# Output products of the first expert in 512-token tiles from batch 1 on, with the last 64 tokens of each batch gathered in DRAM

## What is computed

```
p_packed = sm_attn(p, k, v)                # 32 packed queries per head
out      = sm_attn(q, p_packed, p_packed)  # 576 tokens per batch
x        = out as (4608, 512)
# first expert
xn  = x / sqrt(mean(x*x) + 1e-6) * rms_g
x   = (silu(xn @ w_gate) * (xn @ w_val)) @ w_out       # d_ff 1536
# second expert
h   = x @ w_in
out = (max(h, 0) + alpha * min(h, 0)) @ w_out2         # d_ff 2048
```

## Time and profile before

| | |
|---|---|
| time, median of 3 runs | 1554.76 us (1554.55 to 1554.98) |
| the profiled execution | 1554.32 us |
| its span in the trace | 1552.5 us |
| TensorE busy (matmul) | 1539.6 us, 99% of the span |
| TensorE clock | 0.998 of full |
| VectorE / ScalarE / GpSimd busy | 728.0 / 446.4 / 196.0 us |
| first stage | to 764.8 us; one batch takes 92.3 us |
| second stage | 764.8 to 1552.5 us |

### The profile page before, as it was taken

One profiled execution on the slowest core, in us unless ns is written; L12 is line 12 of the kernel. 1 busy time (PEld: TensorE's weight loads), 2 busy tenths in 40 slices (PEclk: granted clock), 3 DMA queues, 4 the chain that ended last, 5 costly groups with the idle time before them and its releaser, 6 DMA issues.

```text
span 1552.5 us, 25676 instructions
## 1 busy us (share of the span) xinstructions
PE 1539.6 (99%) x10324; PEld 1318.5 (85%) x10324; DVE 728.0 (47%) x1281; ACT 446.4 (29%) x847; POOL 196.0 (13%) x186
## 2 busy tenths in 40 slices
PE   8999999999999999999999999999999999999999
PEld 3889889898988989889988888888888888888887
DVE  5765554645555564655443333333343333333333
ACT  4445344444534444342211111111111111111111
POOL 2700000000000000008551002020201002020000
PEclk9999999999999999999999999999999999999999
DMA  9302111021210302003400001010100000010000
GB/s 354 108 19 79 47 52 61 14 80 46 79 47 13 98 17 77 16 32 136 152 1 28 27 10 44 0 54 0 53 1 27 27 18 36 0 54 0 27 0 27
DMA packets 42738, 76.16 MB, mean 49 GB/s; under 512 B 2208, under 2 KB 19616, under 8 KB 42656
## 3 DMA queue, kind: packets, MB, share of 16 engines
q1 hardware_dynamic: 37760, 66.08, 12.6%
q10 hardware_dynamic: 4896, 8.92, 1.5%
HBM read 56.11 MB, written 18.87 MB: 48 GB/s over the span
## 4 chain that ended last, share of the span: by engine, by line
PE 96%; DVE 3%; ACT 1%; issue 1%; POOL 0%; DVEq 0%; POOLq 0%; ACTq 0%
PE psum L597 30%; PE psum L598 29%; PE psum L599 29%; PE psum L733 3%; PE psum L695 1%; PE psum L635 1%; PE psum L650 1%; PE psum L833 1%; PE psum L683 0%; PE psum L620 0%; PE psum L702 0%; DVE act_sb L1244 0%; DVE h_lo L1247 0%; DVE e L1117 0%; DVE e L1102 0%
## 5 line engine op out<-in xcount | busy, mean ns | idle before, releaser
L1280 DVE TENSOR_TENSOR h_lo<-g,h_hi 128x512 fp32r<-128x512 f32 x144 | 107.4, 746 | 470.3 <-ACT h_hi L1028 470.3
L1028 ACT CAST h_hi<-g 128x512 fp32r<-128x512 f32 x144 | 89.4, 621 | 633.3 <-PE psum L599 598.9
L597 PE MATMUL psum<-an_hi,m_hi 128*128 128x288 f32 x768 | 237.0, 309 | 2.9 <-DVE act_sb L1244 1.4
L597 PE MATMUL psum<-h_hi,ow_hi 128*128 128x288 f32 x768 | 231.6, 302 | 0.6 <-DVE h_lo L1247 0.6
L598 PE MATMUL psum<-an_hi,m_lo 128*128 128x288 f32 x768 | 225.9, 294 | 0.0
L599 PE MATMUL psum<-an_lo,m_hi 128*128 128x288 f32 x768 | 225.8, 294 | 0.0
L598 PE MATMUL psum<-h_hi,ow_lo 128*128 128x288 f32 x768 | 225.8, 294 | 0.0
L599 PE MATMUL psum<-h_lo,ow_hi 128*128 128x288 f32 x768 | 225.8, 294 | 0.0
L597 PEld LDWEIGHTS psum<-h_hi,ow_hi 128*128 128x128 f32 x768 | 144.0, 188 | 26.4 <-issue 25.4
L597 PEld LDWEIGHTS psum<-an_hi,m_hi 128*128 128x128 f32 x768 | 144.1, 188 | 25.3 <-issue 17.0
L1244 DVE TENSOR_TENSOR act_sb<-act_sb,psum 128x288 f32<-128x288 f32 x192 | 85.9, 447 | 168.7 <-PE psum L599 157.2
(11 more groups left out here) (141 smaller groups left out, 2388.7 us busy)
## 6 DMA issues: line engine op xcount, KB each, us to landing
k_sb<-k_t SPq DMA_DIRECT2D x16, 576.0 KB, 5.1
q_sb<-q_t SPq DMA_DIRECT2D x8, 1152.0 KB, 8.7
y_mid<-y_sb SPq DMA_DIRECT2D x16, 576.0 KB, 3.5
xs_raw<-y_mid SPq DMA_DIRECT2D x9, 1024.0 KB, 5.1
out_t<-o_sb ACTq DMA_DIRECT2D x34, 256.0 KB, 2.0
v_sb<-v_s SPq DMA_DIRECT2D x8, 1024.0 KB, 6.6
gv_sb<-w_gv SPq DMA_DIRECT2D x4, 1536.0 KB, 18.8
w_raw_front<-w SPq DMA_DIRECT2D x2, 2560.0 KB, 12.6
```

The costliest lines, as they stand in the source:

```text
L597: nc.tensor.matmul(dst, w_hi, hi, start=start, stop=False)
L1028: nc.scalar.copy(h2_hi[:, f % 2, :], g32[:, f % 2, :]).then_inc(g_hi_done, 1)
L1280: nc.vector.tensor_tensor(h2_lo[:, s, :], g32[:, s, :], h2_hi[:, s, :].bitcast(F32), ALU.subtract).then_inc(g_lo_done, 1)
```

## The change

From batch 1 on a batch is one tile. The up blocks stay 288 wide, but alternate between the halves: block i (0 to 23) is chunk i // 2, half i % 2. The down products of a chunk cover its first 512 tokens at once and are made in two parts of 6 matmuls (output blocks 0, 1, then 2, 3), part by part behind the up blocks, three blocks later (`WIDE_LAG = 3`). High cast and low subtraction are done once a chunk, behind the odd block, 512 wide, in two slots. The 64 tokens that are left of each chunk (of the product in `act_sb`) go by a DMA of their own to the DRAM tensor `rest_mid`, 12 a batch, and the silu of a later odd block waits for that DMA before it writes the slot again. After batch 7 they are loaded again as a ninth tile of 512 tokens (`rest`), split and multiplied (`rest_tile`).

Batch 0 keeps its two halves; the down products of the second are 224 wide (288 less 64). The next batch's `split0` and `split1` move to the end of the tile. Outputs are copied 512 wide to `y_low` and `y_high`, which lie on attention buffers, and stored in two DMAs. SyncE's loop over the batches is unrolled, with the loads of k and v in the middle of a batch. The weight loads of the mid and back part of the second expert wait until the ninth tile is stored. The host reorders the tokens of the result.

```diff
-SLOTS = 3
-LAG = 2
+SLOTS, WIDE_SLOTS = 3, 2
+LAG, WIDE_LAG = 2, 3
...
@@ TensorE
+                for i in range(BLOCKS_OF + WIDE_LAG):
+                    if i < BLOCKS_OF:
+                        up_block(b, i, i // 2, i % 2, at)
+                    if i >= WIDE_LAG:
+                        d, part = (i - WIDE_LAG) // 2, (i - WIDE_LAG) % 2
...
+                        if part == 0:
+                            pe.wait_ge(h_lo_done, h_count(b, d, 0))
+                        down((2 * part, 2 * part + 1), ow_hi[:, d, :], ow_lo[:, d, :], h_hi[:, d % WIDE_SLOTS, :],
+                             h_lo[:, d % WIDE_SLOTS, :], y_ps, d == 0, d == NF1 - 1, out_mm, down_mm,
+                             lambda: at("ready_down", i))
...
@@ ScalarE
+                    for i in range(BLOCKS_OF):
+                        f, half = i // 2, i % 2
...
+                        act.wait_ge(gate_mm, n)
...
+                        elif half == 1 and (b > 1 or f >= WIDE_SLOTS):
...
+                            freed = (b, f - WIDE_SLOTS) if f >= WIDE_SLOTS else (b - 1, NF1 + f - WIDE_SLOTS)
+                            act.wait_ge(rest_out[s], rest_count(*freed))
+                        nc.scalar.activation(act_sb[:, s, half * HALF:(half + 1) * HALF], gate_ps,
+                                             ACT.Silu).then_inc(silu_done, 1)
+                        at("after", i)
+                        if half == 1:
+                            act.wait_ge(h32_done, n)
...
+                            nc.scalar.copy(h_hi[:, s, :], act_sb[:, s, 0:TILE]).then_inc(h_hi_done, 1)
+                        at("between", i)
...
@@ SyncE
+            def store_rest(b, f):
+                i = NF1 + f if b == 0 else 2 * f + 1
+                sp.wait_ge(h32_done, BLOCKS_OF * b + i + 1)
+                src = act_0[:, f % SLOTS, TILE - HALF:HALF] if b == 0 else act_sb[:, f % WIDE_SLOTS, TILE:SEQ]
+                sp.dma_start(rest_mid[:, f, REST * b:REST * (b + 1)], src).then_inc(rest_out[rest_slot(b, f)], 16)
...
+                else:
+                    sp.wait_ge(m_mm, NF1 // 2 * BATCH)
+                    sp.wait_ge(an_lo_done, 2 * BATCH)
+                    load_w2(0, w2_raw_front[:, 0:W2_FRONT // 2, :], 0, W2_FRONT // 2)
+                    sp.wait_ge(y_stored, 32 * (BATCH - 1))
+                    load_w2(1, w2_raw_front[:, W2_FRONT // 2:W2_FRONT, :], W2_FRONT // 2, W2_FRONT)
...
+                for f in range(NF1):
+                    store_rest(b, f)
...
+                if b < BATCH - 1:
+                    store_y(b)
```

More of the change, by code:

```diff
@@ L31 @@
 NT = TOKENS // TILE
+REST = SEQ - TILE
+BLOCKS_OF = 2 * NF1
+assert REST * BATCH == TILE and NT == BATCH + 1
 BANK = 512
@@ L61 @@
     (1, "within", 6): ["means"], (1, "between", 6): ["fold2"], (1, "between", 7): ["newton"],
-    (1, "between", 8): ["fold3"], (1, "within", 10): ["split0"], (1, "between", 10): ["fold4"],
+    (1, "between", 8): ["fold3"], (1, "between", 10): ["fold4"], (1, "after", 11): ["split0"],
+    (1, "between", 11): ["split1"],
 }
@@ L68 @@
     (1, "between", 1): ["fold0"], (1, "between", 3): ["fold1"], (1, "after", 6): ["rsqrt"], (1, "between", 6): ["fold2"],
-    (1, "between", 8): ["fold3"], (1, "between", 9): ["split0"], (1, "between", 10): ["fold4"],
+    (1, "between", 8): ["fold3"], (1, "between", 10): ["fold4"], (1, "after", 11): ["split0"],
+    (1, "between", 11): ["split1"],
 }
@@ L797, in tile @@
[L797 to L812, removed]
@@ L823, in tile @@
[L823 to L828, removed]
+                            pe.wait_ge(y_act, 2)
+                            pe.wait_ge(y_dve, 2)
+                        pe.wait_ge(ow_ready, d + 1)
@@ new lines, in first_tile @@
+                        pe.wait_ge(h_lo_done, h_count(0, d, half))
+                        width = cols.stop - cols.start
+                        down(range(KC), ow_hi[:, d, :], ow_lo[:, d, :], h_hi_0[:, d % SLOTS, 0:width],
+                             h_lo_0[:, d % SLOTS, 0:width], lambda m: y_ps(m)[:, cols], d == 0, d == NF1 - 1,
+                             out_mm if half == 1 else None, down_mm, lambda: at("ready_down", i))
+                    if f < NF1:
+                        at("between", i)
@@ L844, in _ @@
             tiles_of_a(pe, tile, beside)
+            rest_tile()
             lag = 3
@@ L1014, in _, with rest_hi, rest_tile @@
+            def rest_hi(f):
+                if f % 4 == 0:
+                    act.wait_ge(rest_in[f // 4], 16)
+                act.wait_ge(down_mm, h_count(BATCH, f, 0) - 2)
+                nc.scalar.copy(h_hi[:, f % WIDE_SLOTS, :], rest[:, f, :]).then_inc(h_hi_done, 1)
+            def rest_tile():
+                for f in range(1, NF1):
+                    rest_hi(f)
+                out_of_tile(BATCH)
             nc.scalar.preload_act_table_set("natural_log_exp_and_others")
@@ L1235, in beside, with first_tile @@
                     folded(c, int(name[4]), (0, 1) if len(name) == 5 else (int(name[-1]),))
-            def tile(b, half, at):
-                n = 2 * b + half
+            def first_tile(half, at):
                 for f in range(NF1):
-                    s = f % SLOTS
-                    at("within", f)
-                    dve.wait_ge(silu_done, NF1 * n + f + 1)
-                    dve.wait_ge(hidden_mm, NF1 * n + f + 1)
-                    nc.vector.tensor_tensor(act_sb[:, s, :], act_sb[:, s, :], val_ps, ALU.mult).then_inc(h32_done, 1)
-                    at("after", f)
-                    dve.wait_ge(h_hi_done, NF1 * n + f + 1)
-                    nc.vector.tensor_tensor(h_lo[:, s, :], act_sb[:, s, :], h_hi[:, s, :].bitcast(F32),
-                                            ALU.subtract).then_inc(h_lo_done, 1)
-                    at("between", f)
-                    if half == 0 and f == 2 and b > 0:
-                        split(b, 1)
-                dve.wait_ge(y_stored, 16 * n + 16)
-                for m in range(2):
-                    dve.wait_ge(out_mm, (KC - 1) * n + m + 1)
-                    nc.vector.tensor_copy(y_sb[:, m, :], y_ps(m)).then_inc(y_dve, 1)
-                at("end", 0)
@@ new lines, in tile @@
+            def tile(b, at):
+                if b == 0:
+                    for half in range(2):
+                        first_tile(half, at)
+                else:
+                    for i in range(BLOCKS_OF):
+                        f, half = i // 2, i % 2
+                        s, n = f % WIDE_SLOTS, BLOCKS_OF * b + i + 1
+                        dst = act_sb[:, s, half * HALF:(half + 1) * HALF]
+                        at("within", i)
+                        dve.wait_ge(silu_done, n)
+                        dve.wait_ge(hidden_mm, n)
+                        nc.vector.tensor_tensor(dst, dst, val_ps, ALU.mult).then_inc(h32_done, 1)
+                        at("after", i)
+                        if half == 1:
+                            dve.wait_ge(h_hi_done, h_count(b, f, 0))
+                            nc.vector.tensor_tensor(h_lo[:, s, :], act_sb[:, s, 0:TILE], h_hi[:, s, :].bitcast(F32),
+                                                    ALU.subtract).then_inc(h_lo_done, 1)
+                        at("between", i)
+                if b == BATCH - 1:
+                    rest_lo(0)
+                out_of_tile(b)
@@ L1258, in _, with rest_lo, rest_tile @@
+            def rest_lo(f):
+                dve.wait_ge(h_hi_done, h_count(BATCH, f, 0))
+                nc.vector.tensor_tensor(h_lo[:, f % WIDE_SLOTS, :], rest[:, f, :], h_hi[:, f % WIDE_SLOTS, :].bitcast(F32),
+                                        ALU.subtract).then_inc(h_lo_done, 1)
+            def rest_tile():
+                for f in range(1, NF1):
+                    rest_lo(f)
+                out_of_tile(BATCH)
             dve.wait_ge(consts_set, 4)
```

321 lines of the change are left out of this document (221 added, 100 removed).

## The result

| | before | changed |
|---|---|---|
| time, median (lowest to highest of 3 runs) | 1554.76 us (1554.55 to 1554.98) | 1569.16 us (1567.49 to 1570.20) |
| ratio of the runs, 95% interval | | 1.0091 [1.0068, 1.0114] |
| profiled execution / its span | 1554.32 / 1552.5 us | 1567.49 / 1565.7 us |
| one batch, batches 1 to 6 | 92.32 us | 89.37 us |
| batch 7 to the start of stage two | 78.89 us | 112.05 us (with the ninth tile) |

What follows compares the result with a forecast made beforehand. TensorE, busy 99% of the span, was taken to bound the kernel. Terms -8.3 + 10.5 + 1.8 + 1.5 + 5.0 - 1.4 = +9.1 on 1554.3 gave 1563.4, forecast as 1564 us, range 1552 to 1572.

Steps and rivals of the forecast that it cites:

- The price of the columns: Down products of all batches and the ninth tile: fewer, wider matmuls change the time by -8.3 us in sum.
- The rival that priced 512 at 0.234: Down products: 512 wide costs its columns at the 288 price, the 8.3 us gain disappears, 1572 us; chance 0.02.
- The beginning of a batch: Up blocks 2 and 3, batches 1 to 7: new waits for silu and multiply, 1.5 us each, +10.5 us.
- The exponentials ... are covered by this very wait: Beginning of a batch: the wait at up block 3 hides the exponentials of the next block but one, no added cost.
- The middle of a batch: Block 13's gate part waits for the silu of block 12, 0.3 us in batches 1 to 6, +1.8 us.
- Other tight places: Shorter down steps make just-in-time waits late: 0.2 us a batch and 0.3 for batch 0, +1.5 us.
- The stores: 64-token pieces: free in batches 0 to 6; in batch 7 queued behind weight loads, delaying block 5's silu, +5.0 us.
- the rival in which all batches queue: Stores of pieces land 2 us late in each of batches 1 to 6, 12 us more, 1570 to 1576 us; chance 0.13.
- The stall that goes: Last half of batch 7: TensorE's wait for a low subtraction beside GpSimd's weight split disappears, -1.4 us.
- only the columns count: Whole kernel: short waits don't appear and stores land early, 1545 us; with partial waits up to 1551, chance 0.12.

Runs made afterwards that it cites:

- all three edits: Changed kernel with fold5 early, exponentials one block later, and batch 7's weight loads behind pieces 1 and 5: 1550.57 us, ratio 0.9968 to the kernel before.
- the exponentials alone: Changed kernel with the next batch's two exponentials one block later, fold5 left in place: 1565.85 us, ratio 1.0066 to the kernel before.

## Why the prediction was right, and where it was off

The direction and the range held, and the waits that the sum counted are in the trace where it put them. One sentence failed, about the exponentials, and one cost was never thought of, the clock behind the long wait; together they cost 4.4 us, and terms that were counted too high made up a part of it. By the forecast's own steps, against the profiled execution (1554.3 to 1567.5, +13.2 us where +9.1 were summed):

- **The price of the columns** held where rows gave it. In the ninth tile, down blocks start 2.72 us apart, 0.2267 us a matmul. The one width without a row was off: 224 wide, twelve take 1.34 us (127.11 to 128.45), 0.1117 each, where the line gave 0.1045. Batch 0 became 3.2 us shorter and not 3.6. The rival that priced 512 at 0.234 is refuted there. Inside a batch it is half right: a down part that stands alone between two up blocks takes 1.38 us, 0.230 a matmul, where two in a row take 2.72. The Trainium skill (TensorE: Matmul & The Clock Gate, Back-to-back issue gap) gives 2.5 ns over the width at 2.4 GHz for an isolated gap, and 131 ns at 512 for a sustained stream. Neither is what this trace shows, 226.7 ns at 512.
- **The beginning of a batch**: 1.5 us were summed for up blocks 2 and 3. Measured: 2.72 - 1.68 and 1.90 - 1.58, 1.4 in all. Moving `fold5` took this wait away, so its cause is shown; the edit moved ScalarE's and VectorE's part together, so the split between the two is read from the rows.
- **"The exponentials ... are covered by this very wait"** is the sentence that failed. The silu of block 4 still came late: the down part before block 5 took 1.87 us instead of 1.38, 0.5 a batch, and moving the exponentials gave 0.6. That is more than the 0.37 by which each batch was longer than forecast (89.37 against 89.0); other terms came out smaller. The slip was to let the wait at block 3 delay TensorE and not ScalarE's own chain: the silu of block 3 waits for block 3's gate part (1.15 us idle, 228.34), so table load, exponentials, wide cast and table load all start later as well.
- **The middle of a batch**: 0.3 were summed. The down part ahead of block 13 took 1.63 or 1.64 us instead of 1.38, 0.25. The silu of block 12 starts 4.71 us after that of block 11 (257.27), where 4.72 were forecast, and block 13 starts when it has ended (262.44). No experiment moves the probabilities' exponential, so this cause is read from the rows and not tested.
- **Other tight places**, 0.2 a batch: down parts take 1.38 us and not 1.36 where they stand alone, about 20 times a batch. That makes 0.4. A batch is 2.3 us longer than its columns would make it (89.37 against 92.3 - 5.3), and 2.1 are named above, so some 0.2 are left for these: something else became shorter by about as much, and it was not looked for.
- **The stores**: the place in the queue, the moment (a piece issued at S + 5.1, landed at about S + 19.8 where 20.5 to 21 were forecast) and the wait on TensorE were right; 3.9 us idle instead of 5.0. What was missing is its consequence: the block behind the wait ran at half clock, 3.01 us instead of 1.58. Together 5.5 us, and 5.6 came back when the loads were moved. Elsewhere the pieces cost nothing even when stored twice, so the rival in which all batches queue is refuted.
- **The stall that goes** went: in the changed kernel no long subtraction (the longest is 2.38 us) stopped TensorE in batch 7. That a lag of three is what protects it is shown by the lag of two, where three of them did.
- The execution profiled also reached its first up block 0.9 us later than that of before (34.49 against 33.55). In the seven experiments it is between 33.94 and 34.62, always later than in the one trace of before, and I don't know why.

So the four parts that differ from the forecast are 2.1 us in batches 1 to 6, 0.8 in batch 7, 0.4 in batch 0 and 0.9 at the start, 4.2 where 4.1 were to be found. The first two are in the main the exponentials (3.0 in six batches) and the half clock (1.4), less what the beginning of a batch, its middle and the wait for the store fell short of their terms. The last two stay open: traces with the same code there differ by 0.9 us in batch 0 (95.3 and 96.2) and by 0.7 in the start. The medians are 1.2 us further apart than the profiled executions; no trace shows where.

The rival "only the columns count" was refuted as a forecast, but it is nearly where the kernel goes once the order of work is made again: with all three edits it stands at 1550.6 us, 4.5 us under the kernel before, where that rival had 1545. In the trace batch 0 is 3.2 us shorter and six batches 4.7 each, and batch 7 with the ninth tile is 105.3 - 78.9 = 26.4 longer: 4.9 us, of the 8.3 that the columns were to give. A batch still has 0.6 us that the columns don't explain (92.3 - 5.3 = 87.0 against 87.6).

## What to carry to other kernels

Wider tiles are worth the fixed part of each matmul that disappears, here 10 ns (288 wide) to 17 ns (224 wide) by the rows' 0.424 ns a column. With 864 matmuls fewer that was 8.3 us in the whole kernel, and a wait of 1.4 us in each of seven batches is enough to lose it. When a tile's shape or lag changes, write down anew which instruction stands between two dependent blocks, on every engine with a hand-written order, and carry each wait on into the chain of the engine that waits. A small store whose landing frees a buffer should not stand behind megabytes of loads on its queue (here 14.7 us against 1.4); order the loads behind it, where the slack is.

## What the runs showed that was not expected

After TensorE had been idle for 3.90 us in batch 7, the next up block ran at a granted clock of 0.50, 1.2 in place of 2.4 GHz: 3.01 us for 12 matmuls that take 1.58 at full clock. In the two kernels with the weight loads moved, where that wait is absent, the clock over batch 7 and the ninth tile was 1.00. So the wait cost 1.4 us more than itself. In the other experiments the same wait has other lengths. These are the stretches behind it in the runs with a lag of two (3.11 us idle before; with another 0.80 of waiting inside), with `fold5` early (5.05 idle; the up block, then the down part) and with the exponentials alone (3.75 idle; likewise):

```profile
693.68:696.30 2.62, 1.82 (x12) 1.58 (x12) 1.93 (x3) 1.03 (x2) 2.62 (x2) 1.00 0.06 13
...
680.62:683.64 3.02, 3.02 (x12) 3.02 (x13) 1.83 (x2) 1.03 (x2) 3.02 (x2) 0.50 0.05 11
683.64:685.90 2.26, 2.26 (x8) 1.79 (x8) 0.46 (x1) 0.00 (x0) 2.18 (x2) 0.58 0.00 0
...
683.86:686.87 3.01, 3.01 (x12) 3.01 (x13) 2.02 (x2) 1.03 (x2) 3.01 (x2) 0.50 0.05 11
686.87:689.43 2.56, 2.56 (x7) 1.98 (x7) 0.46 (x1) 0.00 (x0) 2.48 (x2) 0.50 0.00 0
```

Behind 3.11 us of idle time the clock stayed at 1.00. Behind 5.05 the slow stretch took in the down part too (2.26 us instead of 1.38, 2.3 us lost in all), and behind 3.75, a shorter wait, the down part was slower still (2.56, 2.6 lost). So the length of the wait alone doesn't give its price.

A matmul 224 wide costs 0.1117 us, 0.02 less than one of 288, where 64 columns at the price between 288 and 512 would be 0.027. So the line through 288 and 512 doesn't reach down to 224: by it the fixed part is 17 ns there and 10 ns at 288.
